# Attention with the probabilities as the stationary operand and the values, widened by columns of ones, as the moving one

## The reference

```python
mask = q_assign[:, :, :, None] == k_assign[:, :, None, :]
scores = scale * np.matmul(q, k.transpose(0, 1, 3, 2))
scores = np.where(mask, scores, -1000000000.0)
scores = scores - np.max(scores, axis=-1, keepdims=True)
attn = np.exp(scores)
attn = attn / (np.sum(attn, axis=-1, keepdims=True) + 1e-09)
return np.matmul(attn, v).astype(np.float32)
```

## Time and profile before

| | |
|---|---|
| median of three runs | 971.63 us |
| the profiled execution | 973.64 us |
| its span, first to last instruction | 971.8 us |
| mean granted TensorE clock | 0.939 of full speed |
| TensorE busy with matmuls | 880.1 us (91%) |
| VectorE, ScalarE, GpSimd busy | 513.0, 293.4, 225.8 us |
| part 4, the chain that ended last | PE 80%, DVE 11%, issue 6% |

### The profile page before, as it was taken

How to read it: one execution, slowest core, us unless ns; L and a number is a source line. 1 busy time by engine, 2 the same in 40 slices (tenths; PEclk the granted TensorE clock), 3 DMA queues, 4 the chain that set the end, 5 groups by cost and what they waited for, 6 DMA issues and landing times.

```text
span 971.8 us, 11830 instructions
## 1 busy us (share of the span) xinstructions
PE 880.1 (91%) x4205; PEld 620.6 (64%) x4206; DVE 513.0 (53%) x683; ACT 293.4 (30%) x558; POOL 225.8 (23%) x175
## 2 busy tenths in 40 slices
PE   5799989999899989509999999969999999999998
PEld 2455555555445554207777777757888888888886
DVE  4667888777888755626566665534321311131111
ACT  3133333333333334503434444423121211121111
POOL 6045655655665442150000000020000100000000
PEclk9579999988999989858999999988999999999999
DMA  4122222222221121366555555652000200010001
GB/s 123 50 70 67 71 68 75 73 78 72 75 67 48 48 82 60 140 222 237 199 199 204 202 196 206 211 183 74 0 1 1 87 1 1 0 44 1 1 1 43
DMA packets 41105, 86.93 MB, mean 89 GB/s; under 512 B 4216, under 2 KB 10584, under 8 KB 41056
## 3 DMA queue, kind: packets, MB, share of 16 engines
q1 hardware_dynamic: 39136, 79.99, 25.4%
q0 software_dynamic: 1920, 6.29, 1.9%
HBM read 60.53 MB, written 17.83 MB: 81 GB/s over the span
## 4 chain that ended last, share of the span: by engine, by line
PE 80%; DVE 11%; issue 6%; DMA 1%; ACT 0%; SPq 0%; DVEq 0%; POOL 0%; ACTq 0%
PE bank L1414 7%; PE bank L1415 7%; PE bank L1416 7%; PE bank L1214 4%; PE pair L1161 4%; PE bank L1354 3%; PE first_pair L1345 3%; PE first_pair L1346 3%; PE first_pair L1347 3%; PE bank L1355 3%; PE bank L1356 3%; PE first_pair L1199 3%; PE first_pair L1201 3%; DVE has_tmp L890 2%; PE bank L1131 2%
## 5 line engine op out<-in xcount | busy, mean ns | idle before, releaser
L1088 DVE TENSOR_TENSOR g_sb<-bank,a_sb 128x512 f32<-128x512 f32 x36 | 24.9, 692 | 196.7 <-PE bank L1416 196.7
L1414 PE MATMUL bank<-x_hi,wt 128*128 128x512 f32 x288 | 115.0, 399 | 1.4 <-DVE x_lo L1057 1.4
L1415 PE MATMUL bank<-x_lo,wt 128*128 128x512 f32 x288 | 114.6, 398 | 0.0
L1416 PE MATMUL bank<-x_hi,wt 128*128 128x512 f32 x288 | 114.5, 398 | 0.0
L844 DVE TENSOR_REDUCE neg_max<-pair 128x1 f32<-128x768 f32 x93 | 88.5, 951 | 45.8 <-PE pair L1161 45.7
L346 POOL TENSOR_TENSOR prob_sum<-prob_sum,prob 128x768 f32<-128x768 f32 x56 | 102.5, 1831 | 11.6 <-ACT prob L582 9.6
L959 DVE TENSOR_TENSOR wt<-w_raw,wt 128x2048 fp32r<-128x2048 f32 x41 | 92.9, 2287 | 10.2 <-ACT wt L661 9.8
L582 ACT ACTIVATE prob<-first_pair 128x384 f32<-128x384 f32 x128 | 59.6, 486 | 83.7 <-PE first_pair L1201 56.6
L1214 PE MATMUL bank<-prob,v_sb 128*64 128x384 f32 x384 | 83.8, 520 | 0.0
L1161 PE MATMUL pair<-kc,qb 96*128 96x384 f32 x186 | 61.7, 417 | 6.1 <-DVE neg_max L844 5.2
L1414 PEld LDWEIGHTS bank<-x_hi,wt 128*128 128x128 f32 x288 | 54.6, 190 | 15.1 <-DVE x_lo L1057 1.8
(11 more groups left out here) (212 smaller groups left out, 1666.1 us busy)
## 6 DMA issues: line engine op xcount, KB each, us to landing
w_raw<-in_moe_w_dram SPq DMA_DIRECT2D x32, 1024.0 KB, 5.2
x_slots<-zeros SPq DMA_DIRECT2D x10, 512.0 KB, 3.7
x_slot<-x_slots SPq DMA_DIRECT2D x18, 256.0 KB, 4.0
y_slots<-y_sb SPq DMA_DIRECT2D x16, 256.0 KB, 4.5
q_raw<-in_q_dram SPq DMA_DIRECT2D x16, 192.0 KB, 2.4
k_raw<-in_k_dram SPq DMA_DIRECT2D x16, 192.0 KB, 2.5
v_sb<-in_v_dram SPq DMA_DIRECT2D x16, 192.0 KB, 2.3
qb<-qa SPq DMA_DIRECT2D x16, 192.0 KB, 2.6
```

The source lines that it names most:

```text
L1414: pe.matmul(to[:, :], w[0], x2_hi[:, kk, :], start=(kk == 0), stop=False)
L1415: pe.matmul(to[:, :], w[0], x2_lo[:, kk, :], start=False, stop=False)
L1416: last = pe.matmul(to[:, :], w[1], x2_hi[:, kk, :], start=False, stop=(kk == KD - 1))
```

## The change

The stationary operand of `times_v` is now a 128x128 block of `prob` (keys by queries), and the moving one is `v` with 66 columns: 64 of the values and two of ones. A key tile takes six float32 matmuls of 66 columns instead of two of 384. The result stands with the queries on the partitions, six pieces of 66 columns in one bank, and the column of ones gives each query's sum. So `add_probs`, `unit1("sum")`, `denominators`, `take_out` and `unit1("out")` are gone, and `token_major` reads the bank directly, now as VectorE's first work of a round. Its semaphore `o_taken`, not ScalarE's, frees the bank.

```diff
-        v_in_sb = [sba(f"v_sb{i}", [P, NT, D], F32) for i in range(4)]
+        v_in_sb = [sba(f"v_sb{i}", [P, NT, VW], F32) for i in range(4)]
+        o_tiles = o_ps[:, 0:NT * VW].rearrange("p (t w) -> p t w", w=VW)
@@ the loads of v
-                sp.dma_start(v_in_sb[u][:], v_heads[n].rearrange("p (t d) -> p t d", t=NT)).then_inc(v_in[u], 16)
+                sp.dma_start(v_in_sb[u][:, :, 0:D], v_heads[n].rearrange("p (t d) -> p t d", t=NT)).then_inc(v_in[u], 16)
@@ GpSimd, a round
-                pool_adds = valid(r) and r < DVE_ADDS
-                if pool_adds:
-                    add_probs(pool, link, r, 1)
-                    add_probs(pool, link, r, 2)
                 if valid(r - 1):
                     fill_lost(r - 1)
-                if pool_adds:
-                    add_probs(pool, link, r, 3)
                 for n in split(r):
                     low_parts(n)
-                if pool_adds:
-                    add_probs(pool, link, r, 4)
-                    add_probs(pool, link, r, 5)
@@ ScalarE
                 if j == 0 and n >= 2:
                     act.wait_ge(o_full, n - 1)
-                    act.wait_ge(psum_ready, n - 1)
-                if p4: take_out(r - 1)
@@ VectorE
+            for u in range(4):
+                dve.memset(v_in_sb[u][:, :, D:VW], 1.0)
-                dve.wait_ge(t1_full, t1_index["out", n] + 1)
+                dve.wait_ge(o_full, n + 1)
                 dve.wait_ge(found_ready, n + 1)
...
+                link(dve.tensor_scalar(den[:], o_tiles[:, :, D], 1e-9, None, ALU.add))
+                link(dve.reciprocal(rden[:], den[:]))
+                link(dve.tensor_tensor(weight[:], rden[:], found[u][:], ALU.mult))
+                xs = x_tok[:, b * NT:(b + 1) * NT, h * D:(h + 1) * D]
+                dve.tensor_tensor(xs, o_tiles[:, :, 0:D], weight[:, :, None].to_broadcast([P, NT, D]),
+                                  ALU.mult).then_inc(o_taken, 1)
@@ VectorE, a round
+                if valid(r - 1): token_major(r - 1)
...
-                if p4: denominators(r - 1)
...
-                if p4: token_major(r - 1)
@@ TensorE
-                pe.wait_ge(exp_done, 12 * n + 2 * j + 2)
...
-                for half in range(2):
-                    last = pe.matmul(o_ps[half * D:(half + 1) * D, 0:HALF], v_in_sb[u][:, j, :],
-                                     prob[s][:, j, half * HALF:(half + 1) * HALF],
-                                     start=(j == 0), stop=(j == NT - 1))
+                for t in range(NT):
+                    if t % 3 == 0:
+                        pe.wait_ge(exp_done, 12 * n + 2 * j + t // 3 + 1)
+                    last = pe.matmul(o_tiles[:, t, :], prob[s][:, j, t * P:(t + 1) * P], v_in_sb[u][:, j, :],
+                                     start=(j == 0 and t == 0), stop=(j == NT - 1), skip_group_check=True)
@@ TensorE, a round
-                if p4: unit1("sum", r - 1)
...
-                if p4: unit1("out", r - 1)
```

More of the change, by code:

```diff
@@ L48 @@
 BIG = float(2 ** 30)
+VW = D + 2
 SCALE = float(D) ** -0.5
@@ L190, in build @@
         prob = [sba(f"prob{i}", [P, NT, S], F32) for i in range(2)]
[L191 to L195, removed]
+        logit_sb1 = sba("logit_sb1", [3 * C, S], F32)
+        den = sba("den", [P, NT], F32)
+        rden = sba("rden", [P, NT], F32)
+        weight = sba("weight", [P, NT], F32)
         v_sum = [sba(f"v_sum{i}", [P, D], F32) for i in range(2)]
@@ L332, in build @@
         for r in rounds:
-            for kind, n in (("max", r + 1), ("sum", r - 1), ("out", r - 1), ("mean", r - 1)):
+            for kind, n in (("max", r + 1), ("mean", r - 1)):
                 if 0 <= n < HEADS:
@@ L338, in valid @@
             return 0 <= n < HEADS
[L340 to L351, removed]
         block = whole.enter_context(nc.Block())
@@ L512, in fill_lost @@
                                         lost[u][:, :, None].to_broadcast([P, NT, D]), ALU.mult))
-                pool.wait_ge(t1_free, t1_index["out", n] + 1)
+                pool.wait_ge(o_taken, n + 1)
                 xs = x_tok[:, b * NT:(b + 1) * NT, h * D:(h + 1) * D]
@@ L587, in unit0 @@
                 at, full, free, base = operand_bank(n)
-                logits_to = prob_sum if n == 1 else logit_sb
+                logits_to = logit_sb1 if n == 1 else logit_sb
                 act.wait_ge(full, base + unit + 1)
@@ L598, in unit0 @@
                 ins.then_inc(free, 1)
[L600 to L604, removed]
             def v_means(n):
@@ L809, in centroids_in @@
                 dve.tensor_copy(en_t[:], bank[0][:, P:P + KD * E].rearrange("p (k e) -> p k e", k=KD)).then_inc(setup_dve, 1)
[L811 to L815, removed]
             def unit0_odd(n, unit):
@@ L902, in _ @@
             for r in rounds[2:]:
-                p4, steady = valid(r - 1), r != -3
+                steady = r != -3
+                if valid(r - 1): token_major(r - 1)
                 if r == -1:
@@ L919, in _ @@
                 if r == -2: mask_rows(1)
[L920 to L924, removed]
-                if p4: token_major(r - 1)
+                for t in early_tile(r, 0): keep_turned(t, pair[:, t % 2, :])
                 for n in masked(r)[:1]: row_max(n, 1)
@@ L936, in _ @@
                 for n in masked(r)[:1] if r >= 0 else []: row_max(n, 5)
[L937 to L940, removed]
+                for place in (1, 2):
+                    for t in early_tile(r, place): keep_turned(t, pair[:, t % 2, :])
             for j in range(NT, TT):
@@ L1121, in unit0 @@
                 at, full, free, base = operand_bank(n)
-                logits_of = prob_sum if n == 1 else logit_sb
+                logits_of = logit_sb1 if n == 1 else logit_sb
                 if base + unit > 0:
@@ L1171, in unit1 @@
                     last = pe.transpose(t1[0:NT, 0:P], neg_max[n % 2][:], ident)
-                elif kind == "sum":
-                    pe.wait_ge(psum_ready, n + 1)
-                    for half in range(2):
[L1175 to L1183, removed]
                 else:
```

14 lines of the change are left out of this document (1 added, 13 removed).

## The result

The changed kernel takes 944.01 us in the median of four runs (941.73 to 948.75); the kernel before, on the same chip, 969.39 (966.73 to 979.37). The ratio is 0.975, with a 95% interval of 0.971 to 0.979. The profiled execution took 944.68 us with a span of 942.8, 29.0 us less than the span before.

The account below looks back on a forecast made before the run. TensorE was taken as nearly the only bound of the attention. A full-clock round went 21.16 - 3.65 + 3.9 = 21.4; with clock, start and end, -6.4 us in all gave 966 us, own range 954 to 979, likely range 945 to 991.

Parts of the forecast that it names:

- sums: TensorE's sums over partitions in each attention round go: 0.77 us a round less.
- turns: TensorE's six turns in each attention round go: 1.28 us a round less.
- waits for VectorE, gone: TensorE's waits in a round: 1.0 of 1.34 us for den, 0.5 for a maximum, 0.1 for ScalarE go.
- the price of the tile: A key tile of the product, twelve instructions, takes 1.45 us where it took 0.79: +0.65 a tile, 3.9 a round.
- The clock: With the wait for den cut to 0.35 us, TensorE keeps the full clock throughout, from about 65 us on.
- rival 2: TensorE's clock falls in steady rounds without idling: 986 us as often as now (0.11), 1014 once a round (0.10).
- +5.0: Round 0 has no sum or turns to lose and starts at the lower clock: +5.0 us in all.
- The end: Round 13 gives -4.0 us, rounds 14 and 15 +3.7, and the stretch after the last head -3.9.
- What hides: VectorE's first work of a round, ScalarE's output copy, v's smaller loads and start fills: nothing charged, or 0.3 us for fills.
- Contention: VectorE's has_tmp, held up by GpSimd's additions at 1.55 us, falls to 0.2 us as five additions a head go.
- rival 1: The product's tile takes 1.2 us, or TensorE waits counted as work go too: 24 us less, 942; chance 0.15.
- Rival 3: In the product, loads and streaming take turns: 0.66 us more a tile, 63 in all, 1029 us; chance 0.06.

Follow-up runs that it names:

- a_wait_turns: a_wait with six turns of constants behind its added wait, and a wait for their bank: 987.82 us, ratio 1.019 against the kernel before.
- a_order: The changed kernel with TensorE's calls reordered, so that more lies between the pieces of unit0 that share a bank: 938.66 us, ratio 0.970 against the kernel before.
- b_one_add: The kernel before with one of GpSimd's five additions a head left, heads 0 to 13, sums wrong by that: 929.32 us, ratio 0.959.
- a_wait: The changed kernel with TensorE also waiting for VectorE's first row maximum ahead of unit0's third piece: 953.58 us, ratio 0.985 against the kernel before.
- a_adds_back: The changed kernel with five additions a head given back to GpSimd on buffers nobody reads: 944.03 us, ratio 0.975 against the kernel before.
- a_wide: The changed kernel with 18 columns of ones in place of 2, so 82 columns move: 940.46 us, ratio 0.972 against the kernel before.
- a_single_early: a_single with VectorE's copy of the values made one round earlier and the order of a_order: 909.43 us, ratio 0.937 against the kernel before.
- a_single: The changed kernel with probabilities and a copy of the values in F32R, one load a matmul, less exact: 915.63 us, too scattered for a ratio.
- b_den_first: The kernel before with VectorE's copy of the sums moved ahead of find_keys, every addition kept: 938.53 us, ratio 0.969.

## Why the prediction was wrong

By its steps, for a round at the full clock:

| term | forecast | by the runs |
|---|---|---|
| sums | -0.77 | -0.77 (from the same rows) |
| turns | -1.28 | -1.28 (a_wait_turns: 22.19 - 20.91) |
| waits for VectorE, gone | -1.6 | -2.24 |
| wait that is new | (0.35 left in the row above) | +0.30 |
| six tiles, with what they do to the groups behind | +3.9 | +2.87 (what is left) |
| round, from 21.16 | 21.4 | 20.04 |

- **The step that failed is the price of the tile,** "1.32 + 0.13 = 1.45", "+0.65 a tile, 3.9 a round". It came to 2.87, that is 0.48 a tile, and over 16 heads the 1.03 us a round make 16 of the 23 us by which the sum was short. (By a_order, which has no wait, the term is 19.96 - 18.92 + 0.77 + 1.28 = 3.09, and its share 13.) The 0.11 for a load was right, and so was the bound by loads. Wrong was the 0.13 ahead of the first load: the mean of 1.33 is twelve loads and nothing else. That alone, at the low end of the 1.32 to 1.58 that I allowed, is 6 x 0.12 = 0.7 us a round. And the tile of before cost more than its 0.79: the loads of what follows did not start until it was nearly over. TensorE's loads (PEld), of the kernel before:

```profile
205.59 0.20 PEld L1214 LDWEIGHTS bank<-prob,v_sb 128*64 128x64 f32 x4
206.38 0.31 PEld L1131 LDWEIGHTS bank<-cst,q_split 128*128 128x128 f32 x3 [0.60 <-DVE has_key L888]
206.86 0.20 PEld L1214 LDWEIGHTS bank<-prob,v_sb 128*64 128x64 f32 x4 [0.17 <-issue]
```

  The product's four loads are over at 205.79, and `q_split`'s first starts 0.60 us later, when the last of the four matmuls is nearly done. The `has_key` in the brackets is not the cause: it was over at 205.87, and the same 0.60 stands behind every tile of this round, also ahead of a score that waits for nothing (at 201.34). In the changed kernel `q_split`'s load stands right behind the product's twelve:

```profile
235.09 1.42 PEld L1156 LDWEIGHTS bank<-v_sb,prob 128*128 128x128 f32 x12
236.37 0.36 PEld L1084 LDWEIGHTS bank<-cst,q_split 128*128 128x128 f32 x3
```

  So what follows passes faster: from the start of `q_split` to that of the next tile it takes 236.81 - 236.48 = 0.33 us where it took 206.86 - 206.38 = 0.48 by the loads of both. The tiles alone would add 8.0 - 6 x 0.80 = 3.2; the round against that of b_one_add gives 2.87 (20.04 - 0.30 - 18.92 + 0.77 + 1.28), so the groups behind the six tiles give back some 0.3 (0.1 by a_order). That the 64-wide tiles held the next load back is read from these rows; the two forms differ in the moving columns too, 384 and 66, and no run varied either by itself.
- **The waits.** I left 0.35 us for a piece of `unit0`, and 0.30 is there, with VectorE's copy as the cause. But the waits that went were larger by 0.4 than those that the timeline prints. The round of b_one_add gives their sum; the rows of one round don't. Over twelve rounds this makes 4 of the 23 us.
- **The clock** was right where it was costed: full throughout the rounds, worth (264.05 - 12 x 21.16) = 10 us. The 17 us that rival 2 gave for the falls in rounds 1 to 12 don't agree with that, and the "about six stretches" from which they would decide against the change is too many: by 3.4 us each, two would have eaten the forecast's gain. The cause of the falls was only half right: I named the wait alone, and a_wait and a_wait_turns show that in this round it took the turns as well. At the start it was wrong. The clock was to be full "from about 65 us on"; it is from 54, and the kernel before gets there at 61. Windows of 1 us, of before and of the changed kernel:

```profile
60.00:61.00 1.00, 1.00 (x7) 1.00 (x6) 0.78 (x1) 0.36 (x1) 0.00 (x0) 0.80 0.10 25
61.00:62.00 1.00, 1.00 (x8) 0.97 (x8) 0.28 (x1) 0.90 (x3) 0.00 (x0) 1.00 0.78 172
```

```profile
53.00:54.00 1.00, 1.00 (x13) 0.69 (x12) 0.45 (x1) 0.26 (x1) 0.00 (x0) 0.80 0.78 204
54.00:55.00 1.00, 1.00 (x10) 0.91 (x9) 1.00 (x2) 0.00 (x0) 0.00 (x0) 1.00 0.02 3
```

  Of the 5.4 us between +5.0 and -0.4 this is about (61 - 54) / 2 = 3.5, an estimate. The cheaper tile explains part of the rest. Why the clock rises earlier no run tested, and since this mark moves by 5 us between kernels of nearly the same work, this part of the miss may be chance.
- **The end:** rounds 13 to 15 and the tail gave -6.0 where -4.2 was forecast, again the tile.
- **What hides** held, for TensorE waits for none of it in the list above: VectorE's new first work, ScalarE, the fills, and the loads of `v` in small pieces, which take 3.0 us for 2.3 and delay nobody.
- **Contention.** `has_tmp` fell to 0.208 us as forecast, and it is worth 0.13 us a round here by a_adds_back. In the kernel before the additions were worth 18.92 against 21.16, but a moved call got more than half of that (19.90).

The outcome is rival 1's in size (942) and only partly in cause. It named waits that count as work, and those went. But its tile was to take 1.2 us and takes 1.33, so that the size came out is in part luck. It was given 0.15. Rival 2's clock falls didn't come; a_wait_turns shows them in eleven stretches. There 34 us come on top of a_wait, of which thirteen rounds of turns are 13 x 1.3 = 17, and the falls the other 17: 1.5 a stretch, less than half of the 3.4 that I had priced from longer ones. Rival 3, loads and streaming in turn, falls by the tile of 1.33 us where it had 1.32 + 0.66, and by a_wide: 16 more columns a matmul change a round by nothing. The Trainium skill's rule that stood beside it (TensorE: Matmul & The Clock Gate, Part 3) doesn't hold in this kernel.

The other half of the story is what the change is worth. In rounds without waits the old form takes 18.92 and the new 20.04 - 0.30 = 19.74 (19.96 in a_order): the product with stationary probabilities costs at least 0.8 us a round more than what it replaces, since 12 loads of 128 columns stand for 4 of 64. The 25 us by which the changed kernel is faster came from the waits and clock falls that it also removed, and one moved call gets as much without it.

## What to carry to other kernels

Before a costly operation is replaced, remove the wait beside it: here one call moved on VectorE gave 32 us in the medians, and the new product alone, by 0.8 us in each of 16 rounds, would have cost 13. Price rows of small float32 matmuls by their loads, count the wait against a version of the kernel that has none, and look at whether what follows can load early. Where the clock falls, look at what runs right behind the idle time, and not only at its length. And compare kernels from a mark behind the start: here the start alone moved by 5 us.

## What the runs showed of the hardware

- Idle for 1.2 us on TensorE left the clock at 2.4 GHz in every round; the same idle time with six float32 turns behind it brought 1.2 GHz in nearly every round (953.6 against 987.8 us, of which about half is the turns' own time). Other kernels fell without such turns: behind waits of 1.38 and 1.08 us in a_single_early, and near 166 us in a_single with none over 0.67.
- A row of float32 matmuls with 128x128 stationary and 66 or 82 columns moving takes 0.11 us an instruction either way; with `F32R`, of one instruction each, half as long a matmul. Six bf16 matmuls with a 128x128 stationary operand took 0.17 us together.
- Behind the product in two 64-column halves, with 384 columns moving, the next group's load started 0.60 us late; behind the 128-column one, with 66 moving, at once.
- Beside GpSimd's additions VectorE's operation of 0.207 us took 1.55, 1.32 and 0.92 us in the median (before, b_den_first, a_adds_back). Before the change that came with rounds of 21.16 in place of 18.92; in a_adds_back with rounds only 0.13 us longer.
